# Gram products in half fills over eight steps, and the last eight rounds of each inverse on VectorE

## The chip, the cores and the metric

One core of one Trainium2 chip runs the whole program in one launch. The metric is the device time in microseconds. The engines are named as the profile names them: PE is TensorE (PEld its weight loads), DVE is VectorE, ACT is ScalarE, POOL is GpSimd, SP issues most transfers.

## The reference

The inputs are q, k, v of shape (4, 8, 768, 48) and beta of shape (4, 8, 768), all f32. A delta rule runs over the 768 positions, and its output goes through two feed-forward layers.

```python
k_n = k / (norm(k) + 1e-06)
for t in range(768):
    y[:, :, t] = q[:, :, t] @ state
    v_old = state.T @ k_n[:, :, t]
    state = state + beta[t] * outer(k_n[:, :, t], v[:, :, t] - v_old)
x = y as (3072, 384)
h = x @ w_in;  x = (cubic(h) / quadratic(|h|)) @ w_out     # w_in 384x2048, w_out 2048x384
h = x @ w_in2; out = (h * tanh(softplus(h))) @ w_out2
```

## The kernel before

The change is in the first part, the delta rule (`delta_rule`), which takes about the first 296 us of the span; the feed-forward part behind it is not touched. The 768 positions are cut into T = 6 **tiles** (`tau`, or `j` where a later tile is prepared), each of 4 chunks `c` of 32 positions. The four batches lie in four blocks of 32 partitions, and the eight heads are taken in two groups `g` of four. A tile is so walked in NQ = 8 **steps**, s = 2c + g. The two groups are independent chains: step s needs the state that step s - 2 left.

In each step PE issues, in this order: `solve` (L389, hz_ps, the inverse times the residual z), perhaps a Gram fill (L359, side_ps), `q_state` (L402, y_bank), `k_state` of the next step (L376, ks_ps), `turn_y` of the step before (L445), `update` (L416, st_bank), `within` (L430, y_bank). DVE issues `updates` (L675, u_blk, needs hz_ps; PE's `update` needs it), `residual` of the next step (L664, z, needs ks_ps), the work for later tiles, and `copy_low` (L681, state, needs `update`). ACT copies the other half of the state, copies y and scales v.

A tile needs, before its first solve, the inverse of a unit triangular 32 x 32 matrix per head and block. It is prepared two tiles ahead:

- the **Gram fills**: four per tile, 32 products each, f = 0 to 3, all into the one bank side_ps from tile 2 on. Fill f waits until DVE has read fill f - 1 (`gram_used`). DVE's `scale_gram` (L627, L628) turns a fill into n_mat and p_mat; it needs the tile's weights (`root_inverse` and `weights`, eight small operations, L591 to L610). In tiles 1 to 3 the fills of tile tau + 2 stand in steps 0 to 3, in tile 0 in steps 1 to 4.
- `turn_n` (L645): DVE transposes n_mat in two halves, behind the last fill.
- `rounds` (L201, L204): 31 rounds, r = 31 down to 1, each a product and a subtraction on r x (32 - r) elements per partition, each operation waiting for the one before. DVE makes all of tile 0's, in 62 operations at the start; POOL makes all of tiles 1 to 5, and then raises `inv_ready`.
- `turn_x` (L654): at a tile's end DVE transposes the inverse into x_mat, behind `copy_low` of step 7 and `spread_w` (L636). The first solve of the next tile waits for it.

At each tile's start PE first waits for `inv_ready` and makes `keep_warm(BURST)` (L342): twelve 128x512 bf16 products of a zeroed tile, whose result nobody reads, while DVE makes `turn_x`. SP waits for `st_done` of the second group of a chunk, then issues the load of kv_run for the next tile and of kq for tile tau + 3.

Of the kernel before, what the change touches and what calls it, by code (L numbers as in the profile page):

```python
# [13 lines left out]
C = 32  # L14
# [7 lines left out]
NQ = CT * G2  # L22
# [4 lines left out]
BURST = 12  # L27
EARLY = 20
TOK = B * CT * C
DM = HEADS * D  # L30
# [8 lines left out]


LATE = [(0, i, i - NP // 2 + 1) for i in range(NP // 2, NP)]
SWAP = [(1, i, NP + 3 + i) for i in range(NP)]


def build(nc, kq_t, kv_n, beta_n, consts, w1, w2, coef, out):

    x1 = nc.dram_tensor("x1_dram", (DM, T, TOK), F32).ap()
    x2 = nc.dram_tensor("x2_dram", (DM, T, TOK), F32).ap()
    with ExitStack() as ctx:
        w = Weights(nc, ctx)  # L50
        hand = Handover(nc, ctx)
        delta_rule(nc, kq_t, kv_n, beta_n, consts, x1, w1, w, hand)
        w.allocate(nc, ctx, "late")
        feed_forward(nc, x1, x2, w1, w2, coef, out, w, hand)


# [49 lines left out]
def delta_rule(nc, kq_t, kv_n, beta_n, consts, x1, w1, w, hand):  # L106

    with ExitStack() as ctx:
# [82 lines left out]

        STEPS = 2 * (C - 1)

        def rounds(eng, tt, j, own, step, done, first, last):
# [35 lines left out]
        def _(sp):  # L230
# [46 lines left out]
            for tau in range(T):  # L277
                if tau == T - 1:
                    for i in range(2, NP // 2):
                        w.load(sp, w1, i)  # L280
                if tau and tau + 3 < T:
                    load_norm(tau + 3)
                for c in range(CT):
                    if tau + 1 < T:

                        sp.wait_ge(st_done, index(tau, c, 1) + 1)
                        load_kv(tau + 1, c)
                    if tau + RING < T:
                        for r in range(HALVES):
                            load_kq(sp, tau + RING, c, r)  # L290
                    if c == 0 and tau:
                        store_y(tau - 1, 1)
                    if c == 2:
                        store_y(tau, 0)
                if tau == 2:
                    for cp in range(2):
                        sp.wait_ge(hand.y_stored[cp], 16 + 16)
                    hand.load_x(sp, x1, 0)
# [5 lines left out]
        def _(pool):  # L304
# [20 lines left out]
            for j in range(1, T):  # L325
                if j >= 2:
                    blank(j)
                pool.wait_ge(n_turned_ready, TURNS * (j + 1))
                rounds(pool, nc.gpsimd.tensor_tensor, j, 0, pool_step, STEPS * (j - 1), C - 1, 0)
                pool.sem_inc(inv_ready, 1)  # L330

        @block.tensor
        def _(pe):
# [9 lines left out]

            def gram_fill(j, f):

                cp, r = f // 2, f % 2
                if r == 0:
                    for c2 in range(2):
                        pe.wait_ge(kq_loaded[slot(j, 2 * cp + c2)], 32 * (j // RING) + 32)
                if j >= 2:  # L350

                    pe.wait_ge(gram_used, 4 * j + f)
                by_event()
                fill = fill_of(bank_of(j, f))
                for c2 in range(2):
                    for s in range(G2 * V):
                        for b in range(B):
                            both = kq[rows(r), slot(j, 2 * cp + c2), :, B * s + b, :]
                            last = nc.tensor.matmul(fill[quad(b), :, c2, s // V, s % V], both[:, 0], both,  # L359
                                                    start=True, stop=True)  # L360
                last.then_inc(gram_done, 1)

# [98 lines left out]
            for tau in range(T):  # L461
                for s in range(NQ):
                    c, g = s // G2, s % G2
                    q = index(tau, c, g)
                    fill = s - (1 if tau == 0 else 0)
                    if tau and s == 0:
                        pe.wait_ge(inv_ready, tau)
                        if tau + 1 < T:
                            pe.wait_ge(gram_used, 4 * (tau + 1) + 4)
                        by_event()  # L470
                        keep_warm(BURST)
                    solve(tau, c, g)
                    if tau + 2 < T and 0 <= fill < 4:
                        gram_fill(tau + 2, fill)
                    q_state(tau, c, g)
# [94 lines left out]
        def _(dve):  # L570
# [68 lines left out]
            def turn_n(j, a, b):  # L639

                dve.wait_ge(gram_used, 4 * j + 4)
                if j >= 3:
# [3 lines left out]
                                    ).then_inc(n_turned_ready, 1)  # L646

            def turn_x(j, a, b):

# [60 lines left out]
            for tau in range(T):  # L710
                for s in range(NQ):
# [7 lines left out]
                    if (tau, s) == (0, 1):  # L719
                        root_inverse(2)  # L720
                    if fill == 0 and tau + 2 < T:
                        weights(tau + 2)
                    if tau + 2 < T and 0 <= fill < 4:
                        scale_gram(tau + 2, fill)
                    if s == (5 if tau == 0 else 4) and tau + 3 < T:
                        root_inverse(tau + 3)
                    copy_low(tau, c, g)
                    if (tau, s) == (0, 0):
# [3 lines left out]
                    if fill == 2 and tau + 3 < T:  # L732
                        sums(tau + 3, half_n, CG)
                    if fill == 3 and tau + 2 < T:
                        turn_n(tau + 2, 0, half_k)
                    if fill == 4 and tau + 2 < T:
                        turn_n(tau + 2, half_k, C)
                    if s == 7 and tau + 1 < T:
                        spread_w(tau + 1)
                    if s == NQ - 1 and tau + 1 < T:  # L740
                        turn_x(tau + 1, 0, half_k)
                        turn_x(tau + 1, half_k, C)
# [445 lines left out]
```

## Time and profile before

| | |
|---|---|
| median of 3 runs | 1146.16 us (1144.45 to 1147.41) |
| the profiled execution | 1137.16 us, its span 1135.4 us |
| first solve of tiles 0 to 5 | 56.02, 98.93, 143.51, 190.28, 231.11, 262.71 us |
| busy over the span | PE 1029.8 us, DVE 869.6, ACT 779.8, POOL 227.7 |
| mean granted PE clock | 0.953 |

The tiles' starts are the starts of PE's L389 behind each L342. The profiled execution is 9 us below the median of the runs that were not profiled.

### The profile page before, as it was taken

The page shows a single profiled execution, that of the slowest core. Times are in us where ns is not written, and L with a number is a line of the kernel's source. Part 1 is how long each engine was busy: PE and PEld are TensorE (multiplying, and loading weights), DVE is VectorE, ACT ScalarE, POOL GpSimd, SP SyncE. Part 2 cuts the span into 40 slices and gives each one's busy share as a digit, 9 for nine tenths or more (in the row PEclk, how much of TensorE's full clock was granted, in tenths as well). Part 3 has the DMA queues.
Part 4 walks back from the last instruction along what each step waited for, and adds up shares of the span by engine and source line. Part 5 has one row for each costly group of instructions (what it writes and reads, how often), then busy time and mean ns, then how long its engine had stood idle before and what let it go on. Part 6 is the DMA issues. An engine that isn't in the chain of part 4 may idle for free.

```text
span 1135.4 us, 24237 instructions
## 1 busy us (share of the span) xinstructions
PE 1029.8 (91%) x10274; PEld 819.1 (72%) x10280; DVE 869.6 (77%) x948; ACT 779.8 (69%) x991; POOL 227.7 (20%) x380
## 2 busy tenths in 40 slices
PE   4478788898778999999999998899999999999997
PEld 2366566666657788777787776778888888888886
DVE  4965646565389888788887877999787878888885
ACT  1143524465488998999998897987676767676764
POOL 5088887780010001001001000000000000000000
PEclk7588979899889999999999999999999999999999
DMA  7823434232343343524324353530100101010000
GB/s 176 238 59 103 114 99 128 73 88 98 101 91 77 74 112 63 123 55 112 74 55 111 74 147 89 136 111 1 56 1 10 45 0 56 0 56 1 29 1 28
DMA packets 35104, 86.99 MB, mean 77 GB/s; under 512 B 4416, under 2 KB 12096, under 8 KB 35008
## 3 DMA queue, kind: packets, MB, share of 16 engines
q1 hardware_dynamic: 27584, 59.13, 17.3%
q0 software_dynamic: 6912, 25.17, 11.6%
q10 hardware_dynamic: 512, 1.31, 0.5%
q8 instruction: 73, 1.20, 0.4%
q14 instruction: 23, 0.19, 0.1%
HBM read 46.27 MB, written 14.16 MB: 53 GB/s over the span
## 4 chain that ended last, share of the span: by engine, by line
PE 33%; DVE 20%; ACT 12%; issue 6%; DMA 1%; ACTq 0%; DVEq 0%; POOLq 0%
PE o_ps L854 6%; PE o_ps L856 6%; PE o_ps L855 6%; PE h_ps L854 5%; PE h_ps L856 5%; PE h_ps L855 5%; DVE val L1078 5%; DVE den L1035 5%; ACT rec L942 4%; DVE pa L1041 4%; ACT rec L950 3%; DVE val L1062 2%; ACT pa L918 2%; DMA val<-pa 1%; DVE den L1069 1%
## 5 line engine op out<-in xcount | busy, mean ns | idle before, releaser
L854 PE MATMUL o_ps<-g_hi,w_hi_early 128*128 128x512 f32 x288 | 115.5, 401 | 21.8 <-DVE g_lo L1084 15.7
L931 ACT ACTIVATE g_hi<-val 128x1024 fp32r<-128x1024 f32 x96 | 101.9, 1062 | 42.5 <-DVE val L1078 36.8
L845 POOL DMA_DIRECT2D val<-pa x48 | 41.5, 864 | 427.4 <-DVE pa L1041 427.4
L854 PE MATMUL o_ps<-g_hi,w_hi_late 128*128 128x512 f32 x288 | 114.4, 397 | 8.8 <-DVE g_lo L1084 8.3
L1062 DVE TENSOR_TENSOR val<-val,rec 128x1024 f32<-128x1024 f32 x96 | 117.0, 1219 | 5.6 <-DMA val<-pa 5.6
L1078 DVE SCALAR_TENSOR_TENSOR val<-den,val 128x1024 f32<-128x1024 f32 x96 | 117.4, 1223 | 5.0
L1084 DVE SCALAR_TENSOR_TENSOR g_lo<-val,g_hi 128x1024 fp32r<-128x1024 f32 x96 | 117.7, 1226 | 2.0 <-ACT g_hi L931 2.0
L855 PE MATMUL o_ps<-g_lo,w_hi_early 128*128 128x512 f32 x288 | 113.5, 394 | 0.0
L856 PE MATMUL o_ps<-g_hi,w_lo_early 128*128 128x512 f32 x288 | 113.3, 393 | 0.0
L855 PE MATMUL o_ps<-g_lo,w_hi_late 128*128 128x512 f32 x288 | 112.9, 392 | 0.0
L856 PE MATMUL o_ps<-g_hi,w_lo_late 128*128 128x512 f32 x288 | 112.8, 392 | 0.0
L854 PE MATMUL h_ps<-x_hi,w_hi_early 128*128 128x512 f32 x288 | 112.4, 390 | 0.3 <-ACT den L923 0.3
L855 PE MATMUL h_ps<-x_lo,w_hi_early 128*128 128x512 f32 x288 | 112.2, 390 | 0.0
L856 PE MATMUL h_ps<-x_hi,w_lo_early 128*128 128x512 f32 x288 | 112.1, 389 | 0.0
L856 PE MATMUL h_ps<-x_hi,w_lo_late 128*128 128x512 f32 x288 | 112.0, 389 | 0.0
L854 PE MATMUL h_ps<-x_hi,w_hi_late 128*128 128x512 f32 x288 | 112.0, 389 | 0.0
L855 PE MATMUL h_ps<-x_lo,w_hi_late 128*128 128x512 f32 x288 | 112.0, 389 | 0.0
L950 ACT ACTIVATE rec<-rec 128x1024 f32<-128x1024 f32 x96 | 101.1, 1053 | 1.5
L925 ACT ACTIVATE den<-h_ps 128x1024 f32<-128x1024 f32 x48 | 49.3, 1027 | 65.9 <-PE h_ps L856 65.9
L1069 DVE SCALAR_TENSOR_TENSOR den<-den,rec 128x1024 f32<-128x1024 f32 x48 | 58.8, 1224 | 42.7 <-ACT rec L950 42.7
L201 POOL TENSOR_TENSOR inv_t<-n_turned,inv 128x31 f32<-128x31 f32 (+15 forms) x155 | 78.0, 503 | 58.0 <-DVE n_turned L645 40.0
L204 POOL TENSOR_TENSOR inv<-inv,inv_t 128x31 f32<-128x31 f32 (+15 forms) x155 | 86.9, 560 | 12.2
(114 smaller groups left out, 2179.7 us busy)
## 6 DMA issues: line engine op xcount, KB each, us to landing
val<-pa POOLq DMA_DIRECT2D x48, 512.0 KB, 4.6
w_raw<-w SPq DMA_DIRECT2D x16, 768.0 KB, 5.1
kv_run<-kv_n SPq DMA_DIRECT2D x24, 384.0 KB, 3.7
x_raw<-x_dram SPq DMA_DIRECT2D x12, 768.0 KB, 5.7
kq<-kq_t SPq DMA_DIRECT2D x44, 192.0 KB, 4.7
x_dram<-stage SPq DMA_DIRECT2D x12, 384.0 KB, 4.3
x_dram<-stage SPq DMA_DIRECT2D x6, 768.0 KB, 4.1
out<-stage SPq DMA_DIRECT2D x5, 768.0 KB, 4.1
```

What stands on the lines that cost most here:

```text
L201: tt(prod, n_turned[:, j % 2, r, 0:r].unsqueeze(2).broadcast_to(shape), inv[:, j % 2, r:r + 1, r:C].broadcast_to(shape), ALU.mult).then_in ...
L204: tt(inv[:, j % 2, 0:r, r:C], inv[:, j % 2, 0:r, r:C], prod, ALU.subtract).then_inc(step, 1)
L854: nc.tensor.matmul(dst, hi, rhs_hi, start=first, stop=False)
L855: nc.tensor.matmul(dst, hi, rhs_lo, start=False, stop=False)
L856: return nc.tensor.matmul(dst, lo, rhs_hi, start=False, stop=last)
L931: act_fn(g_hi[:, n % 2], val[:, n % 2], ACT.Copy, scale=-1.0).then_inc(g_hi_ready, 1)
L950: act_fn(rec[:, e], rec[:, e], ACT.Exp, scale=-1.0).then_inc(rec_ready, 1)
L1035: dve_stt(den[:, e], sq[:, e], cf[:, 6:7], den[:, e], ALU.mult, ALU.add).then_inc(q_ready, 1)
L1062: dve_tt(val[:, e], val[:, e], rec[:, e], ALU.mult).then_inc(ratio_ready, 1)
L1069: dve_stt(den[:, e], den[:, e], ONE, rec[:, e], ALU.add, ALU.mult).then_inc(unit_ready, 1)
L1078: dve_stt(val[:, e], den[:, e], 2.0, val[:, e], ALU.subtract, ALU.mult).then_inc(g_ready, 1)
L1084: dve_stt(g_lo[:, e], val[:, e], -1.0, g_hi[:, e].bitcast(F32), ALU.mult, ALU.subtract).then_inc(g_lo_ready, 1)
```

## The change

Four things are changed.

- A fill can be made in halves: `gram_fill(j, f, chunks)` makes one chunk c2 of it (16 products), the wait for `gram_used` stands before the first half and `gram_done` is raised behind the second. The table GRAM puts one half in each of the eight steps of a tile: fills 2 and 3 of tile tau + 2, then fills 0 and 1 of tile tau + 3. GRAM_0 and GRAM_1 do so for tiles 0 and 1, with two halves in some steps. `weights(tau + 3)` moves from step 0 to step 5 of the tile before, and tile 0's `turn_n(2)` from steps 4 and 5 to step 7.
- POOL makes rounds 31 to 9 of tiles 1 to 5, DVE rounds 8 to 1. Tile 1's stand in a row at the end of tile 0, behind `spread_w(1)`. For tiles 2 to 5 the tables FRONT and BACK put them in steps 5, 6 and 7 of the tile before: round 8 ahead of `copy_low` in step 5, rounds 7 and 6 behind it; 5 ahead and 4, 3 behind in step 6; 2 and 1 ahead in step 7.
- The burst at the start of tiles 2 to 5 goes, with its waits. Tile 1's stays, and starts when half of DVE's sixteen operations are done.
- SP issues the load of kq for tile tau + 3 when `q_state` is done, ahead of the load of kv_run.

```diff
+TAIL = 8
+FRONT = [(), (), (), (), (), (8,), (5,), (2, 1)]
+BACK = [(), (), (), (), (), (7, 6), (4, 3), ()]
+GRAM_0 = ((), ((2, 0, 0), (2, 0, 1)), ((2, 1, 0),), ((2, 1, 1),), ((2, 2, 0), (2, 2, 1)), ((2, 3, 0),), ((2, 3, 1),),
+          ((3, 0, 0), (3, 0, 1)))
+GRAM_1 = (((3, 1, 0), (3, 1, 1)), ((3, 2, 0),), ((3, 2, 1),), ((3, 3, 0), (3, 3, 1)),
+          ((4, 0, 0),), ((4, 0, 1),), ((4, 1, 0),), ((4, 1, 1),))
+GRAM = ((2, 2, 0), (2, 2, 1), (2, 3, 0), (2, 3, 1), (3, 0, 0), (3, 0, 1), (3, 1, 0), (3, 1, 1))
...
+def gram_parts(tau, s):
+    if tau < 2:
+        return (GRAM_0, GRAM_1)[tau][s]
+    ahead, f, c2 = GRAM[s]
+    return ((tau + ahead, f, c2),) if tau + ahead < T else ()
...
                 for c in range(CT):
+                    if tau + RING < T:
+                        sp.wait_ge(q_done, index(tau, c, 1) + 1)
+                        for r in range(HALVES):
+                            load_kq(sp, tau + RING, c, r)
                     if tau + 1 < T:
                         sp.wait_ge(st_done, index(tau, c, 1) + 1)
                         load_kv(tau + 1, c)
-                    if tau + RING < T:
-                        for r in range(HALVES):
-                            load_kq(sp, tau + RING, c, r)
...
-                rounds(pool, nc.gpsimd.tensor_tensor, j, 0, pool_step, STEPS * (j - 1), C - 1, 0)
+                rounds(pool, nc.gpsimd.tensor_tensor, j, 0, pool_step, (STEPS - TAIL_STEPS) * (j - 1), C - 1, TAIL)
...
-                    if tau and s == 0:
-                        pe.wait_ge(inv_ready, tau)
-                        if tau + 1 < T:
-                            pe.wait_ge(gram_used, 4 * (tau + 1) + 4)
+                    if (tau, s) == (1, 0):
+                        pe.wait_ge(dve_step, STEPS + TAIL)
+                        pe.wait_ge(gram_used, 4 * 3 + 1 if tau == 1 else min(4 * (tau + 2) + 2, 4 * T))
                         by_event()
                         keep_warm(BURST)
                     solve(tau, c, g)
-                    if tau + 2 < T and 0 <= fill < 4:
-                        gram_fill(tau + 2, fill)
+                    for j, f, c2 in gram_parts(tau, s):
+                        gram_fill(j, f, (c2,))
...
+            def last_rounds(j, some):
+                for r in some:
+                    if r == TAIL:
+                        dve.wait_ge(inv_ready, j)
+                    rounds(dve, dve_tt, j, 1, dve_step, STEPS + TAIL_STEPS * (j - 1) + 2 * (TAIL - r), r, r - 1)
...
-                    if fill == 0 and tau + 2 < T:
-                        weights(tau + 2)
-                    if tau + 2 < T and 0 <= fill < 4:
-                        scale_gram(tau + 2, fill)
+                    if (tau, s) == (0, 1):
+                        weights(2)
+                    if (tau, s) == (0, 7):
+                        turn_n(2, 0, half_k)
+                        turn_n(2, half_k, C)
+                    if s == (7 if tau == 0 else 5) and tau + 3 < T:
+                        weights(tau + 3)
+                    for j, f, c2 in gram_parts(tau, s):
+                        if c2 == 1:
+                            scale_gram(j, f)
...
+                    if tau and tau + 1 < T:
+                        last_rounds(tau + 1, FRONT[s])
                     copy_low(tau, c, g)
...
+                    if tau and tau + 1 < T:
+                        last_rounds(tau + 1, BACK[s])
+                    if (tau, s) == (0, NQ - 1):
+                        last_rounds(1, range(TAIL, 0, -1))
                     if s == NQ - 1 and tau + 1 < T:
                         turn_x(tau + 1, 0, half_k)
                         turn_x(tau + 1, half_k, C)
```

On DVE, from step 7 of tile 0 to the first solve of tile 1, the order before is this (L675 to L654 are `updates`, `residual`, `copy_low`, `spread_w`, `turn_x`):

```order
L675 TENSOR_TENSOR u_blk<-hz_ps,w_blk 128x768
L664 TENSOR_TENSOR z<-kv_run,ks_ps 128x192
L681 COPY state<-st_bank 48x8x48
L636 TENSOR_TENSOR w_blk<-wgt,blk_mask 128x128
L654 STREAM_TRANSPOSE x_mat<-inv 128x16x32 x2
```

After, the same place holds the two transposes of n_mat, the four operations of `weights(3)` and a `scale_gram` ahead of the copy (the two lines with the lengths 192 are round 8):

```order
L700 TENSOR_TENSOR u_blk<-hz_ps,w_blk 128x768
L689 TENSOR_TENSOR z<-kv_run,ks_ps 128x192
L663 STREAM_TRANSPOSE n_turned<-n_mat 128x512 x2
L622 TENSOR_SCALAR norm<-scratch 128x32
L624 RECIPROCAL scratch<-norm 128x32
L626 TENSOR_TENSOR scratch<-scratch,beta 128x32
L628 TENSOR_TENSOR wgt<-scratch 128x32
L645 TENSOR_TENSOR n_mat<-side_ps,wgt 128x4x64
L646 TENSOR_TENSOR p_mat<-side_ps,upper 128x4x64
L706 COPY state<-st_bank 48x8x48
L654 TENSOR_TENSOR w_blk<-wgt,blk_mask 128x128
L218 TENSOR_TENSOR inv_t<-n_turned,inv 128x192
```

Behind that last row stand the other fifteen operations of rounds 8 to 1, and only then `turn_x`. Before the change nothing of an inverse stood on DVE there.

Also on DVE, steps 5 and 6 of tile 1 after the change (L700 is `updates`, L706 `copy_low`; the row ahead of the first is `residual`):

```order
L218 TENSOR_TENSOR inv_t<-n_turned,inv 128x192
L221 TENSOR_TENSOR inv<-inv,inv_t 128x8x24
L706 COPY state<-st_bank 48x8x48
L218 TENSOR_TENSOR inv_t<-n_turned,inv 128x175
L221 TENSOR_TENSOR inv<-inv,inv_t 128x7x25
L218 TENSOR_TENSOR inv_t<-n_turned,inv 128x156
L221 TENSOR_TENSOR inv<-inv,inv_t 128x6x26
L700 TENSOR_TENSOR u_blk<-hz_ps,w_blk 128x768
L689 TENSOR_TENSOR z<-kv_run,ks_ps 128x192
L218 TENSOR_TENSOR inv_t<-n_turned,inv 128x135
```

Before, in these steps, `updates`, `residual` and `copy_low` followed each other with nothing between. Now a round stands ahead of each copy and two rounds ahead of each `updates`.

On PE, a step of tile 1 from step 4 on has changed from this:

```order
L389 MATMUL hz_ps<-z,x_mat 32x48 x16
L402 MATMUL y_bank<-state,kq 32x96 x8
L376 MATMUL ks_ps<-state,kq 32x96 x8
L445 MATMUL turn_ps<-ident,y_tok 96x128 x2
L416 MATMUL st_bank<-u_blk,kv_run 64x192 x4
L430 MATMUL y_bank<-u_blk,p_mat 32x48 x16
```

to this:

```order
L409 MATMUL hz_ps<-z,x_mat 32x48 x16
L378 MATMUL side_ps<-kq 32x2x32 x16
L422 MATMUL y_bank<-state,kq 32x96 x8
L396 MATMUL ks_ps<-state,kq 32x96 x8
L465 MATMUL turn_ps<-ident,y_tok 96x128 x2
L436 MATMUL st_bank<-u_blk,kv_run 64x192 x4
L450 MATMUL y_bank<-u_blk,p_mat 32x48 x16
```

The half fill (16 products) stands between the solve and `q_state`; steps 1 and 2 of that tile, which held a whole fill, now hold such a half too.

## Rows read from the trace of the kernel before

**Rows 1.** Windows, tiles 1 and 4: us, busy by engine (x), clock, DMA.
```profile
98.93:143.51 44.58, 35.83 (x1133) 26.67 (x1133) 25.59 (x47) 18.23 (x58) 38.72 (x75) 0.92 0.40 110
...
231.11:262.71 31.60, 27.78 (x876) 20.22 (x877) 19.97 (x29) 19.27 (x58) 24.10 (x39) 1.00 0.29 85
```

**Rows 2.** Timeline of PE, one step of tile 4: start, duration, line.
```profile
248.41 0.52 PE L389 MATMUL hz_ps<-z,x_mat 32*32 32x48 f32 x32
...
250.26 0.87 PE L416 MATMUL st_bank<-u_blk,kv_run 128*64 128x192 f32 x8
...
251.43 0.70 PE L389 MATMUL hz_ps<-z,x_mat 32*32 32x48 f32 x32
```

**Rows 3.** Timeline of DVE, the same step, with idle time before.
```profile
248.99 0.96 DVE L675 TENSOR_TENSOR u_blk<-hz_ps,w_blk 128x768 f32<-128x768 f32 x1 [0.28 <-PE hz_ps L389]
...
251.18 0.55 DVE L681 COPY state<-st_bank 48x384 f32<-48x384 f32 x1 [0.90 <-PE st_bank L416]
```

**Rows 4.** Timeline of PE and of DVE, the start of tile 2.
```profile
141.04 2.54 PE L342 MATMUL side_ps<-idle 128*128 128x512 bf16 x11 [0.16 <-issue]
143.51 0.54 PE L389 MATMUL hz_ps<-z,x_mat 32*32 32x48 f32 x32
...
141.13 2.14 DVE L654 STREAM_TRANSPOSE x_mat<-inv 128x512 f32<-128x512 f32 x2
```

**Rows 5.** Timeline of POOL, rounds 31 and 8 of tile 1.
```profile
57.94 0.23 POOL L201 TENSOR_TENSOR inv_t<-n_turned,inv 128x31 f32<-128x31 f32 x1 [40.02 <-DVE n_turned L645]
...
87.01 0.57 POOL L201 TENSOR_TENSOR inv_t<-n_turned,inv 128x192 f32<-128x192 f32 x1
```

**Rows 6.** Timeline of DVE, rounds 8, 7, 5, 4, 2, 1 of tile 0.
```profile
44.42 0.36 DVE L201 TENSOR_TENSOR inv_t<-n_turned,inv 128x192 f32<-128x192 f32 x1
...
45.20 0.34 DVE L201 TENSOR_TENSOR inv_t<-n_turned,inv 128x175 f32<-128x175 f32 x1
...
46.67 0.30 DVE L201 TENSOR_TENSOR inv_t<-n_turned,inv 128x135 f32<-128x135 f32 x1
...
47.33 0.27 DVE L201 TENSOR_TENSOR inv_t<-n_turned,inv 128x112 f32<-128x112 f32 x1
...
48.52 0.22 DVE L201 TENSOR_TENSOR inv_t<-n_turned,inv 128x60 f32<-128x60 f32 x1
...
49.26 0.19 DVE L204 TENSOR_TENSOR inv<-inv,inv_t 128x31 f32<-128x31 f32 x1
```

**Rows 7.** Timeline of DVE: weights(1), then fills scaled.
```profile
51.92 0.19 DVE L604 TENSOR_SCALAR norm<-scratch 128x32 f32<-128x32 f32 x1
...
52.98 0.42 DVE L627 TENSOR_TENSOR n_mat<-st_bank,wgt 128x256 f32<-128x256 f32 x1
...
53.66 0.41 DVE L627 TENSOR_TENSOR n_mat<-st_bank,wgt 128x256 f32<-128x256 f32 x1
```

**Rows 8.** Timeline of POOL and DVE near 102 us; then groups of DVE, 56 to 295.5.
```profile
102.46 0.53 POOL L204 TENSOR_TENSOR inv<-inv,inv_t 128x175 f32<-128x175 f32 x1
...
102.53 0.51 DVE L610 TENSOR_TENSOR wgt<-scratch 128x32 f32<-128x32 f32 x1
...
L610 DVE TENSOR_TENSOR wgt<-scratch 128x32 f32<-128x32 f32 x4 | 1.8, 440 | 0.1
...
L595 DVE TENSOR_TENSOR scratch<-sumsq,scratch 128x32 f32<-128x32 f32 x4 | 0.8, 207 | 0.1
```

**Rows 9.** Timeline of PE, fills and stops: first and last of 13 stops.
```profile
67.39 1.10 PE L359 MATMUL side_ps<-kq 48*32 48x64 f32 x64 [1.69 <-DVE p_mat L628]
...
117.40 0.87 PE L416 MATMUL st_bank<-u_blk,kv_run 128*64 128x192 f32 x8 [1.75 <-DVE u_blk L675]
...
291.77 0.53 PE L402 MATMUL y_bank<-state,kq 128*32 128x96 f32 x13 [1.65 <-issue]
```

**Rows 10.** Windows of 1 us, behind the first and the last stop.
```profile
69.00:70.00 1.00, 1.00 (x25) 0.72 (x18) 0.00 (x0) 0.00 (x0) 0.84 (x3) 0.50 0.13 29
...
293.00:294.00 1.00, 1.00 (x40) 0.68 (x38) 0.24 (x1) 0.57 (x2) 0.00 (x0) 1.00 0.07 16
```

More of the change, by code:

```diff
@@ L192, in delta_rule @@
         STEPS = 2 * (C - 1)
+        TAIL_STEPS = 2 * TAIL
         def rounds(eng, tt, j, own, step, done, first, last):
@@ L342, in keep_warm, with gram_fill @@
                     nc.tensor.matmul(side_ps[:], busy[:, 0:P], busy, start=True, stop=True)
-            def gram_fill(j, f):
+            def gram_fill(j, f, chunks=range(2)):
                 cp, r = f // 2, f % 2
                 if r == 0:
-                    for c2 in range(2):
+                    for c2 in chunks:
                         pe.wait_ge(kq_loaded[slot(j, 2 * cp + c2)], 32 * (j // RING) + 32)
-                if j >= 2:
+                if j >= 2 and 0 in chunks:
                     pe.wait_ge(gram_used, 4 * j + f)
@@ L354, in gram_fill @@
                 fill = fill_of(bank_of(j, f))
-                for c2 in range(2):
+                for c2 in chunks:
                     for s in range(G2 * V):
@@ L360, in gram_fill @@
                                                     start=True, stop=True)
-                last.then_inc(gram_done, 1)
+                if 1 in chunks:
+                    last.then_inc(gram_done, 1)
             def k_state(tau, c, g):
@@ L464, in _ @@
                     q = index(tau, c, g)
-                    fill = s - (1 if tau == 0 else 0)
-                    if tau and s == 0:
-                        pe.wait_ge(inv_ready, tau)
-                        if tau + 1 < T:
-                            pe.wait_ge(gram_used, 4 * (tau + 1) + 4)
+                    if (tau, s) == (1, 0):
+                        pe.wait_ge(dve_step, STEPS + TAIL)
+                        pe.wait_ge(gram_used, 4 * 3 + 1 if tau == 1 else min(4 * (tau + 2) + 2, 4 * T))
                         by_event()
@@ L733, in _ @@
                         sums(tau + 3, half_n, CG)
-                    if fill == 3 and tau + 2 < T:
+                    if tau and s == 3 and tau + 2 < T:
                         turn_n(tau + 2, 0, half_k)
-                    if fill == 4 and tau + 2 < T:
+                    if tau and s == 4 and tau + 2 < T:
                         turn_n(tau + 2, half_k, C)
```

## Prediction, made before the changed kernel was run

> **What bounds the kernel now.** Only the first 296 us are touched, so I read the windows tile by tile, then the timelines of PE, DVE and POOL inside a tile. A tile with Gram fills takes 44.6 us with PE busy for 35.8 of them, one without takes 31.6 with PE busy for 27.8 [rows 1]. In an undisturbed step the solve of one step follows that of the last by 3.02 us (248.41 to 251.43) and PE has no gap in it [rows 2]: PE is the bound there. DVE has room in that step: 0.28 us before `updates` and 0.90 us before `copy_low` [rows 3], and `updates` ends at 249.95, 0.31 us before PE's update at 250.26 [rows 2, 3]. So DVE can take 1.49 us more per step before PE waits. A half fill adds 0.53 us to PE's step (a whole one, 64 records, takes 1.10 with its tail, [rows 9]), so DVE's room grows to 2.02 us there.
>
> At a tile's start PE does not work for the result: DVE makes x_mat in 2.14 us (141.13 to 143.27) and the first solve starts at 143.51, while the burst of 2.54 us lies beside it [rows 4]. POOL is not what is waited for. Its 31 rounds of tile 1 start at 57.94, round 8 at 87.01 [rows 5], and the rest must be made before the tile's end near 96 us. So shortening POOL's part frees nothing by itself. What makes the tiles long beyond the 3.02 us steps are stops of PE and low stretches of its clock. I count 13 stops of 1.5 us or more between 56 and 296 us; the first and the last are [rows 9]. Behind 8 of them the granted clock fell to 0.50, the 1.2 GHz level, as behind the first; behind 5 it did not, as behind the last [rows 10].
>
> **The change part by part**, against the profiled execution of 1137.2 us. "Room" is what DVE can take unseen, as above.
>
> *End of tile 0.* Ahead of the last `copy_low` DVE gets both halves of `turn_n(2)`, at 2.1 us by the pair of x transposes of the same size [rows 4], `weights(3)` at 1.06 (51.92 to 52.98) and one `scale_gram` at 0.68 (52.98, where one starts, to 53.66, where the next does [rows 7]). That is 3.84, less the 0.90 that DVE waits there anyway: 2.9 us late. Then come rounds 8 to 1: 44.42 to 49.45 = 5.0 us, with nothing beside them that PE could use [rows 6]. The burst starts when rounds 8 to 5 are done; the rest (47.33 to 49.45) and `turn_x` give 4.3 us, and twelve products at the lower level take twice the 2.54 us of [rows 4], 5.1: a further 0.7. What DVE is spared in steps 4 and 5 lay in its idle time, so I credit nothing. Sum 8.7 us.
>
> *The same rounds beside POOL.* The trace has the rounds on DVE only where POOL is idle. Small DVE operations beside a working POOL are sometimes held: L610 took 0.51 us at 102.53, ending with POOL's operation of 102.46 to 102.99, where the same kind takes 0.19 as in [rows 6]; over the window its mean is 0.44, that of the like L595 0.21 [rows 8]. The six small groups, of four operations each, lie between 0.02 and 0.25 us above their undisturbed time, 0.11 in the mean. The ends for one operation are 0 and 0.5 (a whole POOL operation); I take 0.11, the mean. For sixteen operations in tile 0: 1.8 us.
> The Trainium skill ("SBUF — State Buffer", Who interferes with whom) says that a VectorE instruction with two SBUF inputs and a GpSimd instruction that reads SBUF exclude each other, and that the later one is held in full. Every round operation is of that kind on both engines. By that rule the upper end would hold for all of them; the row at 102.53 agrees, the one at L595 does not. It is the third rival below.
>
> *Tiles 1 and 2 (POOL at work).* Step 5 gets weights 1.06, a fill scaled 0.68, round 8 at 0.78 (44.42 to 45.20), rounds 7 and 6 at 1.47 (to 46.67) [rows 6, 7]: 3.99, and 0.11 for each of six operations: 4.65 against a room of 2.02, so 2.6 us late. Step 6 gets round 5 (0.66) and 4, 3 (1.19): 1.85 + 0.66 = 2.5, so 0.5. Step 7 gets a fill scaled and rounds 2, 1 (0.93) ahead of a copy with 0.90 of idle time, and the tile's end waits for it: 1.61 + 0.44 - 0.90 = 1.1. Together 4.2 a tile, 8.4.
>
> *Tiles 3 and 4 (no fill, no weights).* Step 5: 2.25 + 0.66 - 1.49 = 1.4; step 6: 2.5 - 1.49 = 1.0; step 7: 0.93 + 0.44 - 0.90 = 0.5. That is 2.9 in tile 3. In tile 4 POOL has done its part and the 0.11 falls away: 0.8 + 0.4 + 0 = 1.2. Sum 4.1.
>
> *Fills.* There are 32 halves before and after, 8 in each of tiles 0 to 3 before. Now they are 10, 10, 8 and 4, and the last two of tile 0 lie beside DVE's late work. PE's part is +0.53 x 2 in tile 1 and -0.53 x 4 in tile 3: -1.1. Against it, in step 2 of tiles 1 and 2 PE waits for DVE's `updates` (1.75 us at 117.40, [rows 9]) and a whole fill lay in that wait; half of it now stands in a later step: +1.1. Sum 0.
>
> *Bursts.* Between x_mat's end and the solve lie 0.24 us [rows 4]; without the burst I take 0.1 less, four times: -0.4 (ends 0 and -1.0).
>
> *The clock.* Without the burst PE stands still for about 2.5 us at the start of tiles 2 to 5. 8 of 13 such stops were followed by a fall, so four more stops give 2.5 falls. A low stretch here lasts 3.4 to 6.9 us and PE's work takes twice as long in it, so one costs 1.7 to 3.4 us. That would be 6.4. Tiles 2, 3 and 5 have a low stretch soon behind their start already, which the new one partly replaces: I take 3.5 (ends -13.6, the four stretches in fill steps gone, and +13.6, four long new ones).
>
> *The load of kq, earlier by the time from `q_state` to `update`.* The half fill of step 5 needs a chunk whose load is issued in step 3. That load lands in about 5 us and the fill comes 6 us later; I take 0.5 (ends 0 and 2). The load of kv_run stands behind it in SP's queue and is needed a tile later.
>
> *What the old stops hide.* PE stops for 1.7 to 2.5 us at the `q_state` of step 7 in tiles 1 to 5, without waiting for an engine (the last is in [rows 9]). In such a stop DVE catches up with what it was late in steps 5 and 6. Over tiles 1 to 4 that gives back at most 8.3 us; I take 6, since step 7's own lateness comes behind it.
>
> Sum: 8.7 + 1.8 + 8.4 + 4.1 + 0 - 0.4 + 3.5 + 0.5 - 6 = 20.6 us. The profiled execution would be 1157.8. It lies 9 us below the median of the runs, and nothing in the change touches what makes that difference, so I forecast 1146.2 + 20.6, rounded 1166 us.
>
> **The rivals.**
> 1. *Faster: the even load keeps the clock up.* Four low stretches stand in the fill steps of tiles 1 to 3 (106 to 113, 150 to 157, 164 to 171, 198 to 205 us), each behind a stop in steps 0 to 2, where fills, weights and sums are crowded on PE and DVE. If half fills leave no stop there, 4 x 3.4 = 13.6 us come back, and with DVE's extra work half hidden (-6 of 12.5) and no new falls (-3.5) the sum is 20.6 - 23 = -2.5, and a stop or two less make it -6: 1140 us. It decides once more than 20 us of low stretches are gone. Against it: most of those stops wait for no engine, so a smoother load does not reach them.
> 2. *Only tile 0's end counts.* The stops hide all that tiles 1 to 4 add, and the clock is as it was: 8.7 + 1.8 - 0.4 = 10 or less, with the chunk of tile 0's work in older stops 6: 1152 to 1156 us. For it: PE's gaps make up 9 us of tile 1 [rows 1]. Against it: only one of them lies in steps 5 to 7.
> 3. *Each engine holds the other for whole operations.* 64 operations in tiles 0 to 3 at 0.39 more each: up to +25, some of it hidden: 1180 to 1190 us. It also slows POOL: 23 rounds take 29.1 us [rows 5], with sixteen holds of 0.3 each some 34, which is still below a tile's length, but for tile 2 the inverse starts only some 11 us before tile 1's first solve, and is needed in its step 5, about 20 us behind it. That would make DVE wait there for 2 or 3 us.
> 4. *The change does nothing that can be told:* gains and costs cancel, 1146.
>
> **How the numbers follow.** Forecast 0.54, with a range of its own of 1156 to 1180; rival 1 0.12; rival 2 0.18; rival 3 0.08; rival 4 0.08. A difference of 0.3%, 3.4 us, is about what a measurement of this kernel can tell from none. The sides are: faster 0.12, same 0.08, slower 0.80. The range of 1144 to 1180 leaves out the faster case and most of the third rival.
>
> **What would show it.** In the profile after: DVE's row of round operations (L218, L221) at the end of tile 0 unbroken for 5 to 8 us, with PE idle beside it until the one burst; tile 0 at 52 us or so in place of 42.9. The mean of the 80 such operations on DVE in tiles 0 to 4 beside those of tile 0's start gives the hold: 0.1 us by the forecast, 0.4 by rival 3. `updates` of steps 6 and 7 should have no idle time before them, and PE should wait for u_blk there. At the starts of tiles 2 to 5 PE idles about 2.5 us, with a fall of the clock behind two or three of them. The forecast is wrong if tile 0 is not at least 6 us longer, if PE's waits for DVE in steps 5 to 7 stay under 0.3 us, or if the low stretches shrink from 44 us to under 20.

## The result, and the profile after

The changed kernel takes 1157.53 us (median of 4 runs, 1155.98 to 1158.80), the kernel before, timed beside it, 1145.31 (4 runs); the comparison on record gives a ratio of 1.0127, with a 95% interval of 1.0101 to 1.0154. So it is slower: by 12.2 us by the two medians (their quotient is 1.0107, inside the interval), by 14.5 us by the ratio of 1.0127. The two profiled executions are 19.4 us apart (1137.16 and 1156.54), because that of before was 8 us faster than its own median; where the text below reads terms off the two traces, they add up to about the 19 and not to the 12.

The windows from first solve to first solve, in the columns of [rows 1], here of tiles 0, 1 and 4 after:

```profile
56.10:115.55 59.45, 46.76 (x1193) 33.38 (x1193) 38.40 (x76) 18.06 (x58) 37.66 (x71) 0.68 0.26 76
115.55:163.93 48.38, 33.86 (x1184) 25.79 (x1185) 33.13 (x65) 18.21 (x58) 34.41 (x61) 0.91 0.33 90
...
247.68:281.70 34.02, 27.07 (x864) 20.59 (x865) 24.05 (x45) 19.24 (x58) 14.70 (x21) 0.90 0.26 74
```

Tile 0 has grown from 42.9 to 59.5 us, tile 1 from 44.6 to 48.4, tile 4 from 31.6 to 34.0; tiles 2 and 3 are 1.9 us shorter each; tile 5, up to PE's last `turn_y` (295.4 us before, 316.0 after), is 1.6 longer. Tile 0's sum is the one to look at: DVE's busy time went up by 9 us, and the granted clock down from 0.88 to 0.68.

DVE at the end of tile 0 (timeline: start, duration, line), first, third and last round, then x_mat:

```profile
104.93 0.34 DVE L218 TENSOR_TENSOR inv_t<-n_turned,inv 128x192 f32<-128x192 f32 x1
...
110.50 0.63 DVE L221 TENSOR_TENSOR inv<-inv,inv_t 128x87 f32<-128x87 f32 x1
...
113.06 0.19 DVE L221 TENSOR_TENSOR inv<-inv,inv_t 128x31 f32<-128x31 f32 x1
113.28 2.12 DVE L679 STREAM_TRANSPOSE x_mat<-inv 128x512 f32<-128x512 f32 x2
```

The sixteen operations take 8.32 us (104.93 to 113.25) where tile 0's own took 5.03 [rows 6]. The operation on 128x87 takes 0.63 us in place of 0.25. POOL, in the same moment:

```profile
110.44 0.58 POOL L221 TENSOR_TENSOR inv<-inv,inv_t 128x192 f32<-128x192 f32 x1
111.10 0.56 POOL L218 TENSOR_TENSOR inv_t<-n_turned,inv 128x207 f32<-128x207 f32 x1
```

DVE's operation ends at 111.13, just behind POOL's of 110.44 to 111.02. So do the others: from 106.19 us on, each operation of the row but the last ends 0.05 to 0.20 us behind the POOL operation that was under way when it began.

DVE in steps 5 and 6 of tile 1, and PE's update that waits for it:

```profile
148.28 0.60 DVE L218 TENSOR_TENSOR inv_t<-n_turned,inv 128x192 f32<-128x192 f32 x1
148.92 0.58 DVE L221 TENSOR_TENSOR inv<-inv,inv_t 128x192 f32<-128x192 f32 x1
149.53 0.55 DVE L706 COPY state<-st_bank 48x384 f32<-48x384 f32 x1
150.00 0.32 DVE L218 TENSOR_TENSOR inv_t<-n_turned,inv 128x175 f32<-128x175 f32 x1
...
151.63 0.64 DVE L221 TENSOR_TENSOR inv<-inv,inv_t 128x156 f32<-128x156 f32 x1
152.31 0.96 DVE L700 TENSOR_TENSOR u_blk<-hz_ps,w_blk 128x768 f32<-128x768 f32 x1
```
```profile
153.32 0.87 PE L436 MATMUL st_bank<-u_blk,kv_run 128*64 128x192 f32 x8 [1.95 <-DVE u_blk L700]
```

Neither the copy nor `updates` has idle time before it any more (0.90 and 0.28 us in [rows 3]), and PE stands still for 1.95 us. The same operation in tile 4, when POOL has ended its part (its last operation starts at 263.36), takes 0.35 us:

```profile
268.14 0.35 DVE L218 TENSOR_TENSOR inv_t<-n_turned,inv 128x192 f32<-128x192 f32 x1
```

The start of tile 2, as in [rows 4]; then two windows of 1 us around it, in the columns of [rows 10]:

```profile
163.93 0.86 PE L409 MATMUL hz_ps<-z,x_mat 32*32 32x48 f32 x32 [3.98 <-DVE x_mat L679]
```
```profile
162.00:163.00 1.00, 0.00 (x0) 0.00 (x0) 1.00 (x2) 0.00 (x0) 0.92 (x2) 0.60 0.50 140
164.00:165.00 1.00, 1.00 (x44) 0.88 (x48) 0.15 (x1) 0.00 (x0) 0.92 (x2) 0.50 0.95 336
```

PE idles 4 us there and the clock falls to 0.50. At the starts of tiles 2 to 5 PE waits 3.98, 4.25, 3.38 and 2.24 us for x_mat, and the first solve of each runs at the lower level. At tile 5 the clock had already fallen between 278 and 279 us, before that wait and behind one of 1.38 us for u_blk. The windows of 1 us up to 316 us hold 78 us at the lower level in all, 51 before.

### The profile page after: what moved, and what is told of

Read it like the earlier page. It is cut to its first block, busy times and chain, and to the rows that moved or that the text cites. A ratio compares the mean times of both kernels' runs of the same rounds, so it can differ in the third digit from the quotient of the medians.

```text
span 1154.7 us, 24189 instructions
## 1 busy us (share of the span) xinstructions
PE 1029.5 (89%) x10232; PEld 822.3 (71%) x10232; DVE 900.4 (78%) x1028; ACT 779.3 (67%) x991; POOL 194.0 (17%) x300
## 3 DMA queue, kind: packets, MB, share of 16 engines
q0 software_dynamic: 6912, 25.17, 11.4%
## 4 chain that ended last, share of the span: by engine, by line
PE 33%; DVE 20%; ACT 12%; issue 6%; DMA 1%; ACTq 0%; DVEq 0%; POOLq 0%
PE o_ps L891 6%; PE o_ps L893 5%; PE o_ps L892 5%; PE h_ps L893 5%; PE h_ps L891 5%; PE h_ps L892 5%; DVE val L1115 5%; DVE den L1072 5%; ACT rec L979 4%; DVE pa L1078 4%; ACT rec L987 3%; DVE val L1099 2%; DMA val<-pa 1%; DVE den L1106 1%; ACT pa L955 1%
## 5 line engine op out<-in xcount | busy, mean ns | idle before, releaser
L546 ACT ACTIVATE stage<-turn_ps 96x256 f32<-96x256 f32 x48 | 18.2, 378 | 107.5 <-PE turn_ps L465 107.5
L891 PEld LDWEIGHTS o_ps<-g_hi,w_hi_early 128*128 128x128 f32 x288 | 55.1, 191 | 39.0 <-DVE g_lo L1121 11.7
```

Of the source, the lines that this page charges most:

```text
L891: nc.tensor.matmul(dst, hi, rhs_hi, start=first, stop=False)
```

## The experiments

All times are medians, each beside runs of the kernel before on the same chip; ratios are to that. The kernel before itself moved between 1139.6 and 1145.3 us from one group of runs to the next, so ratios are compared and not times; where an expectation names a time, it is compared as a difference to the kernel before, which stood at 1145 to 1146 us when the first four were written. A difference of two ratios carries some 4 to 5 us of uncertainty (95%). "Low" is the time at the lower clock level from 56 to 316 us in the one profile of each.

**Fills alone.** The changed kernel with the rounds back on POOL.

```diff
-TAIL = 8
-FRONT = [(), (), (), (), (), (8,), (5,), (2, 1)]
-BACK = [(), (), (), (), (), (7, 6), (4, 3), ()]
+TAIL = 0
+FRONT = [()] * 8
+BACK = [()] * 8
...
-                        pe.wait_ge(dve_step, STEPS + TAIL)
+                        pe.wait_ge(inv_ready, 1)
```

> The changed kernel with all 31 rounds of tiles 1 to 5 back on GpSimd; half fills, moved weights and turn_n, no bursts at tiles 2 to 5. Theory (the rounds on VectorE are what costs, 8 us of them at the end of tile 0, held by GpSimd): 1145 to 1150 us, at most 5 over the kernel before; tile 0 about 8 us shorter than in the changed kernel, the waits of TensorE for x_mat at tiles 2 to 5 near 2.3 us each. Rival (the fills, the crowded end of tile 0 and the missing bursts cost through TensorE's clock): it stays above 1154 us.

Measured: 1133.53 us against 1141.21, ratio 0.9927 (0.9900 to 0.9953); low 61 us. It is faster than the kernel before. Neither the theory (up to 5 us slower) nor the rival (above 1154) had that. The rounds on DVE cost 2.0% of the kernel, more than the whole change; something else in the change gives 0.7%. PE waits 2.5 us for x_mat at each of the four starts, as expected.

**Rounds alone.** The kernel before with the same rounds on DVE.

```diff
-                rounds(pool, nc.gpsimd.tensor_tensor, j, 0, pool_step, STEPS * (j - 1), C - 1, 0)
+                rounds(pool, nc.gpsimd.tensor_tensor, j, 0, pool_step, (STEPS - TAIL_STEPS) * (j - 1), C - 1, TAIL)
...
+                    if tau and tau + 1 < T:
+                        last_rounds(tau + 1, FRONT[s])
                     copy_low(tau, c, g)
...
+                    if tau and tau + 1 < T:
+                        last_rounds(tau + 1, BACK[s])
+                    if (tau, s) == (0, NQ - 1):
+                        last_rounds(1, range(TAIL, 0, -1))
```

> The kernel before with rounds 8 to 1 of tiles 1 to 5 on VectorE and nothing else; all bursts stay, whole fills stay in steps 0 to 3. Theory: about 8 us at the end of tile 0 (GpSimd is already at work on tile 2 there, so the sixteen operations take 8 us and not 5) and 1 to 2 us in each of tiles 1 to 4: 1154 to 1160 us. Rival (the clock and the moved fills cost, not the rounds): below 1150 us.

Measured: 1151.84 us, ratio 1.0085 (1.0059 to 1.0111). The 9.7 us are near the lower end of the first theory (8 to 14 over the 1146 of then). From x_mat to x_mat tile 0 is 10.9 us longer than before (its end at 108.38 for 96.55, its first solve 1 us later) and tiles 1 to 4 together 3.9, all of it in tiles 3 and 4 (-0.4, -0.3, +3.3 and +1.3). The row of sixteen takes 10.24 us here (98.11 to 108.35), longer than in the changed kernel. POOL is further on in tile 2's inverse, with longer operations, and even DVE's smallest takes what POOL's takes:

```profile
107.40 0.68 POOL L208 TENSOR_TENSOR inv<-inv,inv_t 128x255 f32<-128x255 f32 x1
107.50 0.62 DVE L205 TENSOR_TENSOR inv_t<-n_turned,inv 128x31 f32<-128x31 f32 x1
```

The same operation takes 0.19 us where POOL is idle.

**Without bursts.** The kernel before without the bursts of tiles 2 to 5.

```diff
-                    if tau and s == 0:
+                    if (tau, s) == (1, 0):
                         pe.wait_ge(inv_ready, tau)
```

> The kernel before without the bursts at tiles 2 to 5 and without the waits ahead of them, nothing else. My prediction's term says +3.1 us (one or two more low stretches of the clock, 0.1 us less at each start): 1148 us. Rival (the bursts only delay the first solve, and the clock falls where it falls anyway): 1143 to 1146.

Measured: 1142.14 us against 1141.21, ratio 0.9995 (0.9970 to 1.0021); low 68 us against 51. No difference can be told. My term of 3.1 us is just outside the interval (2.4 us). The clock did fall at the starts of tiles 2, 4 and 5; at tile 3 it had been low since 184 us.

**Bursts back in the changed kernel.**

```diff
-                    if (tau, s) == (1, 0):
-                        pe.wait_ge(dve_step, STEPS + TAIL)
+                    if tau and s == 0:
+                        pe.wait_ge(dve_step, STEPS + TAIL if tau == 1 else STEPS + TAIL_STEPS * tau)
```

> The changed kernel with a burst at the start of tiles 2 to 5 again, released by VectorE's last round. The profile of the changed kernel has a low stretch of the clock at the start of tiles 2, 3, 4 and 5, each 3.4 to 7 us. If the missing bursts cause them: they go, and the time falls by 4 to 10 us to 1148 to 1153. If not: 1156 to 1158, with the low stretches there as before.

Measured: 1153.32 us, ratio 1.0104 (1.0066 to 1.0143) against 1.0127 of the changed kernel: 2.6 us less, where 4 to 10 were expected, with intervals that overlap. The low stretches at the four starts are gone; the window at the start of tile 2, with PE in the burst and behind it in the first step:

```profile
160.00:161.00 1.00, 0.91 (x9) 0.27 (x10) 0.81 (x1) 0.00 (x0) 0.85 (x2) 1.00 1.00 372
...
162.00:163.00 1.00, 1.00 (x41) 0.84 (x34) 0.51 (x1) 0.00 (x0) 0.84 (x3) 1.00 0.20 66
```

Low fell from 78 to 53 us. That the bursts keep the clock up at a start is shown by these profiles, one of each kernel; that this is worth more than 2 or 3 us is not.

**Tile 1's inverse whole on POOL**, the rest as changed.

```diff
-                rounds(pool, nc.gpsimd.tensor_tensor, j, 0, pool_step, (STEPS - TAIL_STEPS) * (j - 1), C - 1, TAIL)
+                rounds(pool, nc.gpsimd.tensor_tensor, j, 0, pool_step,
+                       (STEPS - TAIL_STEPS) * (j - 1) + (TAIL_STEPS if j > 1 else 0), C - 1, TAIL if j > 1 else 0)
...
-                        pe.wait_ge(dve_step, STEPS + TAIL)
+                        pe.wait_ge(inv_ready, 1)
...
-                    if (tau, s) == (0, NQ - 1):
-                        last_rounds(1, range(TAIL, 0, -1))
```

> The changed kernel with tile 1's 31 rounds all on GpSimd; VectorE keeps rounds 8 to 1 of tiles 2 to 5. Theory (the row of sixteen operations at the end of tile 0 is the largest part of the cost of the rounds, 8.3 us in the trace): 8 to 10 us under the changed kernel, 1148 to 1150 us, and tiles 1 to 4 as long as in the changed kernel. Rival (the rounds in steps 5 to 7 of tiles 1 to 4 cost as much): 3 to 5 us under it, 1152 to 1155.

Measured: 1146.72 us against 1140.11, ratio 1.0064 (1.0040 to 1.0089). Against the changed kernel's 1.0127 that is 0.63%, 7.2 us, a little under the 8 to 10 expected. Against fills alone (0.9927) it is 1.37%, 15.6 us: so by the medians the rounds in steps 5 to 7 of tiles 1 to 4 cost more than the row at the end of tile 0 does, about twice as much, each price within 4 us. The theory had that the wrong way round. In the profiles of these two, tiles 1 to 4 (x_mat to x_mat) are 4.0, 3.4, 1.5 and 1.4 us longer with the rounds, 10.3 in all. Of that, 4.5 are longer waits of PE for x_mat at the starts of tiles 2 to 5 (4.26, 4.33, 3.39 and 2.31 us for 2.48, 2.49, 2.47 and 2.46).

**POOL waits.** POOL starts tile 2's inverse behind DVE's sixteen operations.

```diff
                 pool.wait_ge(n_turned_ready, TURNS * (j + 1))
+                if j == 2:
+                    pool.wait_ge(dve_step, STEPS + TAIL_STEPS)
```

> The changed kernel, but GpSimd starts tile 2's inverse only when VectorE has made its sixteen operations of tile 1. Theory (GpSimd's operations hold VectorE's): those take 5.0 us in a row and not 8.3, tile 0 ends 3.3 us earlier, and the start of tile 2's inverse moves back by 6 us or so, which step 5 of tile 1 can just bear: 1153 to 1156 us. If it was no hold, the sixteen operations still take 8 us and the time rises by 0 to 2 us.

Measured: 1152.45 us against 1140.11, ratio 1.0093 (1.0064 to 1.0123). DVE at the end of tile 0:

```profile
101.76 0.34 DVE L218 TENSOR_TENSOR inv_t<-n_turned,inv 128x192 f32<-128x192 f32 x1
...
105.90 0.25 DVE L221 TENSOR_TENSOR inv<-inv,inv_t 128x87 f32<-128x87 f32 x1
...
107.06 0.19 DVE L221 TENSOR_TENSOR inv<-inv,inv_t 128x31 f32<-128x31 f32 x1
107.29 2.14 DVE L681 STREAM_TRANSPOSE x_mat<-inv 128x512 f32<-128x512 f32 x2
```

The operation on 128x87 is back at 0.25 us, and the row takes 5.49 us: 2.8 less than in the changed kernel, though nothing on DVE was changed. The sixteen durations are those of [rows 6] again; the 0.46 us over 5.03 lie between the operations. So it is POOL's work that holds DVE. The sum of the sixteen durations against that of [rows 6] gives the hold per operation, group by group, in the changed kernel 0.18, 0.22, 0.19, 0.13 and 0.00 us for tiles 1 to 5, and here 0.00, 0.20, 0.19, 0.13 and 0.00: it is nothing in just the two groups beside which POOL does nothing. The time fell by 0.34%, 3.9 us, as expected (1.5 to 4.5), but within intervals that overlap.

**Fills alone with the old loads.** Fills alone, with SP's order as before.

```diff
-                    if tau + RING < T:
-                        sp.wait_ge(q_done, index(tau, c, 1) + 1)
-                        for r in range(HALVES):
-                            load_kq(sp, tau + RING, c, r)
                     if tau + 1 < T:
                         sp.wait_ge(st_done, index(tau, c, 1) + 1)
                         load_kv(tau + 1, c)
+                    if tau + RING < T:
+                        for r in range(HALVES):
+                            load_kq(sp, tau + RING, c, r)
```

> The kernel of the run fills alone (1133.5 us, 0.7% under the kernel before) with the kq loads issued behind the kv_run loads again, as before. If the gain comes from the fills and not from the loads: 1132 to 1137. If the earlier loads shorten TensorE's stops: 1139 to 1143, as the kernel before.

Measured: 1141.86 us against 1140.11, ratio 1.0022 (0.9989 to 1.0054). The gain is gone: it belongs to the loads.

**Tile 0's fills early.** Fills alone, with tile 0 nearly as before.

```diff
-GRAM_0 = ((), ((2, 0, 0), (2, 0, 1)), ((2, 1, 0),), ((2, 1, 1),), ((2, 2, 0), (2, 2, 1)), ((2, 3, 0),), ((2, 3, 1),),
+GRAM_0 = ((), ((2, 0, 0), (2, 0, 1)), ((2, 1, 0), (2, 1, 1)), ((2, 2, 0), (2, 2, 1)), ((2, 3, 0), (2, 3, 1)), (), (),
           ((3, 0, 0), (3, 0, 1)))
...
-                    if (tau, s) == (0, 7):
-                        turn_n(2, 0, half_k)
-                        turn_n(2, half_k, C)
-                    if s == (7 if tau == 0 else 5) and tau + 3 < T:
+                    if s == (6 if tau == 0 else 5) and tau + 3 < T:
                         weights(tau + 3)
...
-                    if tau and s == 3 and tau + 2 < T:
+                    if s == (3 if tau else 4) and tau + 2 < T:
                         turn_n(tau + 2, 0, half_k)
-                    if tau and s == 4 and tau + 2 < T:
+                    if s == (4 if tau else 5) and tau + 2 < T:
                         turn_n(tau + 2, half_k, C)
```

> The kernel of the run fills alone, with tile 0's fills of tile 2 whole in steps 1 to 4, turn_n(2) in steps 4 and 5 and weights(3) in step 6, as near as can be to the kernel before, so that less stands on VectorE at the end of tile 0. In the profile of fills alone tile 0 is 4.5 us longer than in the kernel before. Theory (3.8 us of VectorE's work ahead of the last copy): 3 us less, 1130 us. Rival (that is the clock's chance): 1133 to 1135.

Measured: 1132.32 us against 1140.11, ratio 0.9920 (0.9893 to 0.9946), against 0.9927. Inconclusive: the 0.8 us lie inside the intervals, and so would the 3 us that were expected.

**Loads alone.** The kernel before with the new order of loads, and nothing else.

```diff
+                    if tau + RING < T:
+                        sp.wait_ge(q_done, index(tau, c, 1) + 1)
+                        for r in range(HALVES):
+                            load_kq(sp, tau + RING, c, r)
                     if tau + 1 < T:
                         sp.wait_ge(st_done, index(tau, c, 1) + 1)
                         load_kv(tau + 1, c)
-                    if tau + RING < T:
-                        for r in range(HALVES):
-                            load_kq(sp, tau + RING, c, r)
```

> The kernel before with the kq loads issued at q_state, ahead of the kv_run loads, and nothing else. Fills alone with the old loads gave 1.002 of the kernel before, with the new ones 0.993. If the load order gives the gain by itself (shorter queues ahead of what TensorE needs fetched, so shorter stops): 0.990 to 0.995 here too, 1129 to 1135 us, TensorE's idle time without a releaser clearly under the 28.6 us of the kernel before. If it needs the half fills beside it: 0.998 to 1.002.

Measured: 1130.38 us against 1139.63, ratio 0.9922 (0.9891 to 0.9953). Moving two loads gives 0.8% by itself. The windows of tiles 1 and 4 (the cuts are the starts of the x_mat transposes, not of the first solves):

```profile
98.06:139.77 41.71, 34.32 (x1134) 25.24 (x1133) 24.87 (x48) 18.23 (x59) 36.09 (x72) 0.96 0.41 116
...
221.39:253.95 32.56, 28.11 (x878) 20.32 (x877) 19.97 (x30) 19.38 (x59) 27.93 (x45) 1.00 0.28 76
```

Tiles 1 to 3 take 41.7, 40.8 and 40.9 us (44.6, 46.2 and 41.5 before by the same cuts), tile 4 is 1.0 us longer. But the reason given is not what the profile shows: PE's idle time without a releaser, from 56 to 296 us, is 28.7 us, as before (28.6). The longest stop is 1.9 us for 2.5, and low is 36 us for 51.

**Fills early, with bursts.** The kernel of "tile 0's fills early" with the bursts back.

```diff
-                    if (tau, s) == (1, 0):
-                        pe.wait_ge(inv_ready, 1)
+                    if tau and s == 0:
+                        pe.wait_ge(inv_ready, tau)
```

> The kernel of the run with tile 0's fills early (0.992 of the kernel before: half fills, new load order, all rounds of tiles 1 to 5 on GpSimd), with a burst at the start of tiles 2 to 5 again. Bursts back in the changed kernel gave 0.23% (4 us at the most), bursts out of the kernel before nothing. If they keep the clock up: 1 to 4 us less, 1128 to 1131. If not: 1132 to 1134.

Measured: 1128.50 us against 1139.63, ratio 0.9912 (0.9878 to 0.9946). The lowest ratio of all, but not told apart from loads alone, nor from the same kernel without the bursts (0.9920).

**The kq loads first, but not earlier.** The kernel before; all three loads are issued together.

```diff
                         sp.wait_ge(st_done, index(tau, c, 1) + 1)
+                        if tau + RING < T:
+                            for r in range(HALVES):
+                                load_kq(sp, tau + RING, c, r)
                         load_kv(tau + 1, c)
-                    if tau + RING < T:
-                        for r in range(HALVES):
-                            load_kq(sp, tau + RING, c, r)
```

> The kernel before with the two kq loads ahead of the kv_run load, but all three still issued together, when TensorE's update is done. The load order alone, with kq issued some 1.8 us earlier, gave 0.9922. Theory (three loads of 768 KB in one lump hold up what TensorE has fetched, and parting them by 1.8 us shortens its stops): the lump is as large as before, so 0.997 to 1.003. Rival (kv_run must stand last, or kq first): 0.990 to 0.995.

Measured: 1138.67 us against 1141.16, ratio 0.9993 (0.9967 to 1.0019).

**The kq loads a step later.** The kernel before; kv_run where it was.

```diff
                     if tau + RING < T:
+                        sp.wait_ge(q_done, index(tau, c, 1) + 2)
                         for r in range(HALVES):
                             load_kq(sp, tau + RING, c, r)
```

> The kernel before with the kv_run load where it was and the kq loads issued about 2 us later, at the q_state of the next step. Theory (parting the lump is what helps, whichever part comes first): 0.990 to 0.996. Rival (only kq first or earlier helps): 0.998 to 1.003.

Measured: 1140.78 us against 1141.16, ratio 0.9997 (0.9969 to 1.0025). The order alone gives nothing, and parting the loads the other way round gives nothing. Only kq issued earlier, ahead of kv_run, gives the 0.8%. The theory of the lump of 768 KB falls with this. In these single profiles low is 36 us for loads alone, 68 for kq first and 54 for kq later. Whether the earlier load acts through where PE's stops fall against the clock, or through something that the profile does not list, stays open.

## Why the prediction was right, and where it was not

The forecast was +20.6 us, with 1144 to 1180 as the range; +12.2 was measured, in the direction forecast. It is right as a whole because two wrong terms stand against each other. The runs price its steps as follows (1% is 11.4 us). The four measured prices are differences of neighbours on one path from the kernel before to the changed one, each within 4 to 5 us; that they add up to the whole follows from that and tests nothing:

| step | forecast | measured, from |
|---|---|---|
| fills, crowded end of tile 0, no bursts | +2.9, 0, -0.4, +3.5 = +6.0 | +0.22%, +2.5 us (fills alone with old loads) |
| kq loads earlier | +0.5 | -0.95%, -10.8 us (fills alone, new against old loads); -0.78%, -8.9 us alone |
| rounds in steps 5 to 7 of tiles 1 to 4 | 8.4 + 4.1 - 6 = +6.5 | +1.37%, +15.6 us (tile 1's inverse on POOL, against fills alone) |
| tile 1's rounds at the end of tile 0 | 5.0 + 1.8 + 0.7 = +7.5 | +0.63%, +7.2 us |
| sum | +20.5 | +1.27%, +14.5 us |

**Right: PE and not POOL sets the pace.** Shortening POOL's part freed nothing; with rounds 8 to 1 given back to POOL (fills alone) the kernel got faster.

**Right: the end of tile 0.** The row stands unbroken for 8.3 us, just over what was foreseen (5 to 8), and its price is 7.2 us. The 0.7 of the burst came to nothing: it ended at 114.17, 1.2 us before x_mat did. Tile 0's window grew by 16.5 us, though, more than any term. From the last `residual` to x_mat DVE takes 12.95 us (100.33 to 113.28) for 2.00 before (94.55 to 96.55): 10.95 of it, against 2.9 + 5.0 + 1.8 = 9.7 forecast. The other 5.7 come before that, where the clock was low from 56 to 67 and from 80 to 91 us (mean 0.53 in both windows, 0.84 before). It was low from 97 us on as well. From 56 to 61 us the two programs are still the same on PE. So I take this part for chance, and it is of the same size as the 7 us by which the profiles differ more than the medians. The other traces bear that out for much of it. With the bursts back the program is the same up to the start of tile 2, and there tile 0 takes 59.4 us from x_mat to x_mat, for 63.7 in the changed kernel and 47.1 before. The kernel before without bursts, the same program up to there as the kernel before, takes 50.6. From 56 to 67 us the clock is 0.53 in the changed kernel and 0.84 with the bursts back.

**Right in kind, too small: the hold.** I took 0.11 us per operation, from small operations that met POOL by chance. It is 0.18, 0.22, 0.19 and 0.13 in the four groups beside a working POOL: 11.5 us over 64 operations for 7.0. A chain of such operations on both engines meets at nearly every one, and the two fall into step: most of DVE's then end just behind POOL's, so that one lasts about as long as POOL's and the hold is POOL's time less DVE's own. It fits this that the same sixteen are held by 0.18 in the mean beside POOL operations of mostly 0.37 to 0.60 us, and by 0.27 in rounds alone, beside ones of mostly 0.56 to 0.70. There the smallest is held by 0.43 us, the size of the third rival; in the mean of a row its 0.39 more was too much. It was wrong on POOL: from 105.57 to 110.44 POOL's operations take the same time beside DVE's row as where POOL waits for the row to end (0.53 us on 128x175 in both). One per row does take longer, beside the end of `copy_low` (0.90 us for 0.36 at 104.59). The Trainium skill ("SBUF — State Buffer", Who interferes with whom) says that a VectorE instruction with two SBUF inputs contends with a GpSimd instruction that reads SBUF, and that the ports they share are an exclusive lock. The run in which POOL waits agrees that the two contend: the hold is 0.00 once POOL is still.

**Wrong: "what the old stops hide", -6 us.** The step fails by its credit and by the hold. By the profiles of fills alone and of tile 1's inverse on POOL the tiles grow by 4.0, 3.4, 1.5 and 1.4 us: the forecast without the credit had 4.2, 4.2, 2.9 and 1.2. So little was hidden. In the kernel before with only the rounds added tiles 1 to 4 grew by 3.9 us together, so there most of it was hidden; that the stops did it is not shown. I had read that kernel's room, not that of the changed one, whose loads and fills are elsewhere. The medians say the same: all the rounds together cost 0.85% (9.7 us) on the kernel before and 2.00% (22.8 us) on fills alone, so the parts of this change do not simply add up. Beyond the 10.3 us of the profiles the medians show 15.6, with 4 of uncertainty; the rest is not explained.

**Wrong: the kq loads, +0.5 us.** This is the largest miss. I priced the edit only by whether its fill would wait for it, and kept both ends at 0 and 2; it was worth -9 to -11, each within 4 to 5. Nothing in my sum had a load's issue time as a cause of how long a tile is.

**The clock and the bursts, +3.1 us.** At all four starts PE ran at the lower level, where I had 2.5 of 4 (at tile 5 it had fallen shortly before), and PE idles there 4 us at tiles 2 and 3, 3.4 at tile 4 and 2.2 at tile 5, and not 2.5, since DVE comes late with x_mat at the first three. The bursts back took those stretches away. But in time they are worth 2.6 us in the changed kernel, not clear of noise, and nothing in the kernel before. So a low stretch at a tile's start costs little; that steps there also wait for other things would explain it, but is not shown.

**The first rival** (faster, since the even load keeps the clock up) is refuted: with old loads, even fills give nothing (1.0022), and low was 58 us for 51.

## What to carry to other kernels

Work moved from an engine that nobody waits for to one that PE waits for costs up to its full length there (7.2 us for a row of 8.3), and the length itself can grow when both engines then work on SBUF tiles at once: measure the hold in a row of such operations, not on stray ones. Change one part at a time: here 0.8% of gain from two loads issued earlier was buried under 2% of loss. The version to keep is the kernel before with that one edit (0.9922), or the even fills with it and the bursts (0.9912); the two are not told apart.

## What the runs showed of the hardware

VectorE's tensor_tensor with both inputs in SBUF is held by GpSimd's beside it, by 0.11 to 0.27 us in the mean of sixteen with durations of 0.19 to 0.36 us, and by nothing when GpSimd is idle. In a chain against a chain, VectorE's operation ends just behind GpSimd's: one of 0.19 us took 0.62 beside one of 0.68. The order of three loads of 192, 192 and 384 KB, with the first two issued at `q_state` and not together with the third, was worth 0.8% of the whole kernel; nothing in the page of the profile points to it.
